# Regrouping the attention round of a fused attention, MoE and FFN kernel, with four smaller moves of waits and reads

## The chip, the cores and the metric

The kernel runs on one core of a Trainium2 chip, as one launch. The metric is device time in microseconds, the median of three runs; lower is better. TensorE (PE in the profile) multiplies, VectorE (DVE), ScalarE (ACT) and GpSimd (POOL) work on tiles, and SyncE (SP) only issues DMAs and waits.

## The reference

Three layers follow each other. The first is a gated linear attention over 4 batches of 8 heads, 768 tokens each, head size 48; the second a top-1 mixture of 8 experts; the third a dense layer with an ELU.

```
for t in range(S):                                   # attention, per batch and head
    state = alpha[t][:, None] * state + outer(k[t], v[t])
    y[t] = q[t] @ state
x = y as [3072, 384]
logits = normalised(x) @ normalised(expert_emb).T / tau
e = argmax(logits); gate = softmax(logits)[e]
x = gate * (relu(x @ w1[e]) @ w2[e])                 # w1 384x1024, w2 1024x384 per expert
h = x @ w_in                                         # 384x2048
out = where(h > 0, h, exp(min(h, 0)) - 1) @ w_out    # 2048x384
```

## The kernel before

All engines run side by side, each through its own hand-written list of steps, and each step waits on semaphores for the steps that it needs.

**Attention.** Two heads make a pair, so there are 16 pairs (PAIRS), and round n works on pair n, with parts of the pairs before and behind it. A pair has 6 chunks of 128 tokens, in two halves (0 and 1, three chunks each). `ROUND_PE`, `ROUND_VE`, `ROUND_AC` and `ROUND_PO` are the orders of a round on TensorE, VectorE, ScalarE and GpSimd; `("Tk1", 1)` in round n is the step Tk1 of pair n+1. The steps are:

- TensorE: Ta, Tk, Tq transpose alpha, k and q (three 128x128 each); KT transposes the scaled keys (3 and 2); A is the score product (12 matmuls of 48 rows, in pairs in two row halves of the array); KV the chunk states (20 matmuls with 128x64 weights, in pairs in two column halves); Yi is scores times v (12 per half, weights 128x48); Ys is q times the state (20, weights 48x48, rows and columns halved); YN transposes y and multiplies it with the expert embeddings (6 per half); CT counts tokens per expert (once in four rounds).
- VectorE: G and F are prefix scans over 768 tokens (lines 836 and 844), R a reciprocal between them; Kh and Qh scale keys and queries; M0 masks the scores of half 0; S2 to S5 (line 710) run the state recurrence over the chunks; LA adds logits. The R.., N.. and Y.. names are the router's small steps (argmax, slots, softmax, and the order of the experts), each a chain of its own.
- ScalarE: Kt, C1, Ea, Yn, Ln, yT copy out of PSUM; St1 to St5 copy the chunk states with a scale; SS and SP square x for the norm; Gq is the softmax's Exp.
- GpSimd: M1 masks the scores of half 1 (line 1007), Gm, Za, Zm are small; P0 to P8 are the inverse square root of the norms (lines 959 to 978, "roots"); SC scatters rows of x to DRAM, sorted by expert (line 1015), six per batch; U0 issues the loads of w1 of the second expert (lines 1143 and 1133, 1.5 MB each).

With PPB = 4 pairs per batch, batch b's router steps start in round 4(b+1); the lists `SLOW`, `SOON`, `LAST` hang them behind steps of a round. The last batch (PARTIAL, b = 3) is finished after round 15. PSUM has 8 banks, and each step names the bank that it uses, so the reuse of a bank is a wait.

**Experts.** Rows are processed in 31 tiles of 128 tokens, sorted by expert: XT transposes a tile, M10 and M11 are the two halves of x @ w1 (9 matmuls each), HT transposes h, M2 is h @ w2 (24). ScalarE (Xe, Re, He) and VectorE (Xe, He, Ye) copy and split operands. Tiles 0 and 1 take rows of the first three batches only (EARLY = 2). SyncE waits for all scatters of the last batch before it loads tile 2. `position(t)` reads the expert's number of tile t from `kth` into a register, once in each of M10, M11 and M2. `climb` runs a ladder of small VectorE steps that compute `row`, `kth`, `end_i` (up to n_tiles) and `dst` (to the end).

**FFN.** Six groups of 512 tokens; H is x @ w_in, O accumulates g @ w_out, 16 blocks each; E, M, G, L are the ELU and its split. The output of four tiles per group goes through `of` and four indirect DMAs (line 1406) issued by GpSimd, which also waits for their completion before the program ends.

Of the kernel before, what the change touches and what calls it, by code (L numbers as in the profile page):

```python
# [10 lines left out]
P = 128  # L11
# [59 lines left out]
def build(nc, q, k, v, alpha, emb, tau, w1, w2, w_in, w_out, out):  # L71
# [30 lines left out]
    with ExitStack() as ctx:  # L102
# [138 lines left out]
        for x in (a_at, d_at, e_at, r_at):  # L241
# [56 lines left out]
        ROUTE_PE = [({}, {"Ta0": ("CT",)})] * (BATCHES - 1) + [({"YN1": ("CT",)},)]  # L298
        ROUTE_AC = [({}, {}, {"Ln0": ("Gq",)})] * (BATCHES - 2) + [({}, {"Ln1": ("Gq",)}), ({"Ln0": ("SL0",), "Yn1": ("SL1",), "Ln1": ("Wc", "Gq")},)]
# [22 lines left out]
        def steps_pe(n):  # L322
            out_ = with_route(ROUND_PE, ROUTE_PE, n)
            if n == -1:
                out_ = [("Tk1", 0), ("Ta0", 1), ("Tq0", 0), ("Tq1", 0), ("Ta1", 1)]
            if n in (0, 1):
                out_.insert(place_of(out_, "A0") + 1, ("Tk0", n + 1))
            if n == 0:
                out_.remove(("Tk0", 2))
            return out_  # L330

        def steps_ve(n):
            out_ = with_route(ROUND_VE, ROUTE_VE, n)
# [1297 lines left out]
```

## Time and profile before

| | |
|---|---|
| median of 3 runs | 910.74 us (910.71 to 911.87) |
| the profiled execution | 911.53 us, of which 909.9 us are its span |
| PE busy | 879.2 us (97%) |
| DVE, ACT, POOL busy | 436.1, 320.5, 267.9 us |
| granted TensorE clock | 0.996 of full |

Times in the rows are microseconds from the span's start. The end of a matmul is modelled: a row of three matmuls that starts at 97.95 and lasts 0.49 has its last start some 0.27 (the length of one) before its end. What counts on TensorE is the distance from start to start. A busy TensorE is therefore not a TensorE at its peak. The span falls into attention (0 to 179.3), the hand-over to the experts and the first tiles (to 203.9), the experts (to 475.4, one tile in 9.6), the FFN (to 898.9) and an end without matmuls (to 909.9).

### The profile page before, as it was taken

How to read it: one execution, taken by the hardware profiler on the slowest of the kernel's cores; microseconds unless marked ns; L12 is line 12 of the kernel's file. 1: busy time of each engine (PE TensorE's matmuls, PEld its weight loads, DVE VectorE, ACT ScalarE, POOL GpSimd, SP SyncE). 2: the span in 40 equal slices, each digit the busy share in tenths (PEclk: the TensorE clock that was granted, in tenths of full speed). 3: DMA queues.
4: the chain of work that ended last, by engine and by line, in shares of the span. 5: the costliest groups of instructions: out<-in, count | busy, mean ns of one | idle time of the engine just before them, and what ended most of it. 6: DMA issues, size and time to landing. Idle time of an engine off the chain costs nothing. (4 is left out here: it accounts for less than half of the span.)

```text
span 909.9 us, 16294 instructions
## 1 busy us (share of the span) xinstructions
PE 879.2 (97%) x5725; PEld 777.8 (85%) x5725; DVE 436.1 (48%) x828; ACT 320.5 (35%) x709; POOL 267.9 (29%) x279
## 2 busy tenths in 40 slices
PE   8999999889999999999999999999999999999995
PEld 5787888678989989999888899999999899899894
DVE  7887888872222222322325545445445445445442
ACT  4565646623222222232332223223223223223221
POOL 3114244447545754564807201001001001001001
PEclk9999999999999999999999999999999999999998
DMA  9965774688878789746807102002002002000000
GB/s 155 163 120 116 155 151 96 212 280 268 259 243 280 246 259 302 238 137 189 220 20 235 42 1 70 1 1 70 1 1 70 1 0 70 1 1 35 1 1 35
DMA packets 140975, 107.92 MB, mean 119 GB/s; under 512 B 103354, under 2 KB 129074, under 8 KB 140898
## 3 DMA queue, kind: packets, MB, share of 16 engines
q0 software_dynamic: 25696, 66.09, 22.8%
q1 hardware_dynamic: 115202, 40.79, 20.2%
q8 instruction: 50, 0.82, 0.4%
q14 instruction: 27, 0.22, 0.1%
HBM read 89.51 MB, written 17.35 MB: 117 GB/s over the span
## 5 line engine op out<-in xcount | busy, mean ns | idle before, releaser
L1406 POOL DMA_INDIRECT out<-of,idi x24 | 23.6, 983 | 370.1 <-DVE of L1492 305.4
L1226 PE MATMUL bank<-WX,hdTh 128*128 (+1 forms) x496 | 129.5, 342 | 3.0 <-DVE hdTl L1279 1.7
L1450 PE MATMUL bank<-xT_h,wi_h 128*128 128x512 f32 x288 | 114.3, 397 | 0.0
L1450 PE MATMUL bank<-xT_l,wi_h 128*128 128x512 f32 x288 | 113.7, 395 | 0.0
L1450 PE MATMUL bank<-xT_h,wi_l 128*128 128x512 f32 x288 | 113.5, 394 | 0.0
L1532 DVE TENSOR_SCALAR em<-ee 128x512 f32<-128x512 f32 x96 | 44.7, 465 | 136.0 <-ACT ee L1510 133.8
L1510 ACT ACTIVATE ee<-bank 128x512 f32<-128x512 f32 x96 | 57.3, 597 | 147.2 <-PE bank L1450 144.2
L1212 PE MATMUL bank<-WX,xdTh 128*128 (+1 forms) x372 | 99.7, 403 | 3.3 <-ACT xdTh L1252 1.5
L1513 ACT ACTIVATE g_h<-gg 128x512 fp32r<-128x512 f32 x96 | 60.6, 632 | 116.3 <-DVE gg L1537 114.6
L1150 POOL TENSOR_TENSOR WX<-raw_w,WX 128x3072 fp32r<-128x3072 f32 x14 | 95.5, 6821 | 17.8 <-DMA WX<-moe_w 12.9
L1541 DVE TENSOR_TENSOR g_l<-gg,g_h 128x512 fp32r<-128x512 f32 x96 | 69.9, 728 | 60.2 <-ACT g_h L1513 59.3
L1226 PEld LDWEIGHTS bank<-WX,hdTh 128*128 128x128 f32 x496 | 88.2, 188 | 3.6 <-issue 3.4
L1477 PE MATMUL bank<-wo_h,g_h 128*128 128x384 f32 x380 | 82.6, 339 | 1.2 <-DVEq L423 0.6
L1226 PE MATMUL bank<-WX,hdTl 128*128 (+1 forms) x248 | 83.7, 337 | 0.0
L1212 PEld LDWEIGHTS bank<-WX,xdTh 128*128 128x128 f32 x372 | 67.6, 189 | 18.1 <-issue 4.4
L1477 PE MATMUL bank<-wo_h,g_l 128*128 128x384 f32 x380 | 81.7, 338 | 0.2 <-DVE g_l L1541 0.2
L1477 PE MATMUL bank<-wo_l,g_h 128*128 128x384 f32 x380 | 81.4, 337 | 0.0
L1477 PEld LDWEIGHTS bank<-wo_h,g_h 128*128 128x128 f32 x380 | 68.8, 188 | 10.6 <-issue 1.7
L1258 ACT ACTIVATE hdTh<-bank 128x512 fp32r<-128x512 f32 x62 | 33.8, 596 | 119.8 <-PE bank L1235 119.8
L1537 DVE SCALAR_TENSOR_TENSOR gg<-bank,em 128x512 f32<-128x512 f32 x96 | 66.4, 692 | 3.7 <-DVEq L423 0.5
L1261 ACT ACTIVATE hd<-bank 128x512 f32<-128x512 f32 x62 | 37.0, 598 | 88.5 <-PE bank L1212 88.5
L1477 PEld LDWEIGHTS bank<-wo_h,g_l 128*128 128x128 f32 x380 | 67.3, 189 | 0.5 <-DVE g_l L1541 0.5
(215 smaller groups left out, 1387.2 us busy)
## 6 DMA issues: line engine op xcount, KB each, us to landing
WX<-moe_w POOLq DMA_DIRECT2D x14, 1536.0 KB, 9.9
raw_w<-moe_w POOLq DMA_DIRECT2D x14, 1536.0 KB, 8.6
xd<-sorted_x SPq DMA_DIRECT2D x31, 193.0 KB, 5.3
sorted_y<-yd SPq DMA_DIRECT2D x31, 192.5 KB, 4.6
xg<-sorted_y SPq DMA_DIRECT2D x6, 770.0 KB, 4.4
nat_a<-alpha SPq DMA_DIRECT2D x32, 144.0 KB, 3.3
nat_k<-k SPq DMA_DIRECT2D x32, 144.0 KB, 3.5
nat_q<-q SPq DMA_DIRECT2D x32, 144.0 KB, 3.6
```

The lines of the kernel that those rows point to most:

```text
L1150: po.tensor_tensor(lower[:, cols], raw[x][:, :], upper[:, cols].bitcast(F32), ALU.subtract).then_inc(s_w, 1)
L1212: last = pe.matmul(bank[3 + i][:, :], xdT[t % 2][a][:, k * P:(k + 1) * P], WX[:, bass.ds(off + (b * WE + k * F + i * COLS), COLS)], start= ...
L1226: last = pe.matmul(y_out(t)[:, 0:DM], hdT[a][:, k * P:(k + 1) * P], WX[:, bass.ds(off + (b * WE + KD * F + k * DM), DM)], start=(k == 0 an ...
L1258: return ac.activation(hdT[0][:, cols], bank[1 + i][:, :], ACT.Copy)
L1261: return ac.activation(hd[:, cols], bank[3 + i][:, :], ACT.Relu)
L1450: last = pe.matmul(bank[4 + i % 2][:, :], a[:, k, w], b[:, k, :], start=(k == 0 and m == 0), stop=(k == KD - 1 and m == 2))
L1477: last = pe.matmul(bank[t][:, 0:DM], a[i % 2][:, t * P:(t + 1) * P], b[:, i, :], start=(i == 0 and m == 0), stop=(i == K2 - 1 and m == 2))
L1510: return ac.activation(ee[i % 2][:, :], bank[4 + i % 2][:, :], ACT.Exp)
L1513: return ac.activation(g_h[i % 2][:, :], gg[i % 2][:, :], ACT.Copy)
L1532: return ve.tensor_scalar(em[i % 2][:, :], ee[i % 2][:, :], 1.0, -1.0, ALU.min, ALU.add)
L1537: return ve.scalar_tensor_tensor(out=gg[i % 2][:, :], in0=bank[4 + i % 2][:, :], scalar=0.0, in1=em[i % 2][:, :], op0=ALU.max, op1=ALU.add)
L1541: return ve.tensor_tensor(g_l[i % 2][:, :], gg[i % 2][:, :], g_h[i % 2][:, :].bitcast(F32), ALU.subtract)
```

## The change

The order of the round changes. On TensorE, steps of one kind stand together: `KT0 KT1 Tk1`, then `A0 A1`, then the full-array steps `YN0 Ta0 Ta1 YN1 Tq0 Tq1 Tk0`, then `KV Yi0 Yi1`, `Ys0 Ys1`. KV moves from the fifth place to the thirteenth, and the states St1 to St5 on ScalarE and S2 to S5 on VectorE move to the end of the round. The banks are dealt out anew to allow it. VectorE takes both Kh before M0, and the router's small steps mostly stand behind S5. Squares (SS, SP) and Gq stand in other gaps of ScalarE. All six scatters of batch 2 move to round 14, and the router's steps that they need move too (Rp, Rr, Ng, Nk behind S5 of round 13; Ns, Nt, Nr behind Kh1 of round 14).

After round 15, GpSimd's roots come before U0 ("roots ahead of reads"). VectorE's ladder is cut at n_tiles, and Ye 0 and He 1 stand before its rest. `position` keeps what it read, and a step K reads the next tile's position before HT0. In the FFN, output tiles 0 and 2 go to ScalarE and 1 and 3 to VectorE (before: the other way round), the last group's O14 of tile 3 waits until tiles 0 and 1 of O15 are done, and SyncE waits for the last output scatters in GpSimd's place.

```diff
-        ROUND_PE = (("KT0", 0), ("A0", 0), ("KT1", 0), ("Tk1", 1), ("KV", 0), ("A1", 0), ("Ta0", 2), ("YN0", -1), ("Ta1", 2),
-                    ("Tq0", 1), ("YN1", -1), ("Tq1", 1), ("Tk0", 2), ("Yi0", 0), ("Yi1", 0), ("Ys0", 0), ("Ys1", 0))
-        ROUND_VE = (("G", 1), ("Kh0", 1), ("M0", 0), ("Kh1", 1), ("R", 1), ("S2", 0), ("S3", 0), ("S4", 0), ("S5", 0),
-                    ("F", 1), ("LA", -1), ("Qh0", 1), ("Qh1", 1))
-        ROUND_AC = (("yT0", -1), ("Kt0", 0), ("yT1", -1), ("Kt1", 0), ("St1", 0), ("St2", 0), ("St3", 0), ("St4", 0), ("St5", 0),
-                    ("Ea0", 2), ("Yn0", -1), ("Ln0", -1), ("C1", 0), ("Ea1", 2), ("Yn1", -1), ("Ln1", -1))
+        ROUND_PE = (("KT0", 0), ("KT1", 0), ("Tk1", 1), ("A0", 0), ("A1", 0), ("YN0", -1), ("Ta0", 2), ("Ta1", 2), ("YN1", -1),
+                    ("Tq0", 1), ("Tq1", 1), ("Tk0", 2), ("KV", 0), ("Yi0", 0), ("Yi1", 0), ("Ys0", 0), ("Ys1", 0))
+        ROUND_VE = (("G", 1), ("Kh0", 1), ("Kh1", 1), ("M0", 0), ("R", 1), ("F", 1), ("LA", -1), ("Qh0", 1), ("Qh1", 1),
+                    ("S2", 0), ("S3", 0), ("S4", 0), ("S5", 0))
+        ROUND_AC = (("yT1", -1), ("Kt0", 0), ("Kt1", 0), ("C1", 0), ("Yn0", -1), ("Ln0", -1), ("Ea0", 2), ("Ea1", 2),
+                    ("Yn1", -1), ("Ln1", -1), ("St1", 0), ("St2", 0), ("St3", 0), ("St4", 0), ("St5", 0), ("yT0", 0))
...
-                    out_ += [("U0", 1), ("PM", b)] + roots + [("SC", b * C + j) for j in range(C)]
+                    out_ += [("PM", b)] + roots + [("U0", 1)] + [("SC", b * C + j) for j in range(C)]
                 elif b == PARTIAL - 1 and r == 1:
-                    i = place_of(out_, "M1")
-                    out_[i:i] = roots
-                    out_ += [(f"X{i}", b) for i in range(X_STEPS)] + [("SC", b * C + j) for j in range(HC)]
+                    out_ += roots + [(f"X{i}", b) for i in range(X_STEPS)]
                 elif b == PARTIAL - 1 and r == 2:
-                    i = place_of(out_, "M1") + 1
-                    out_[i:i] = [("SC", b * C + j) for j in range(HC, C)]
+                    out_ += [("SC", b * C + j) for j in range(C)]
...
+        def a_bank(i, h):
+            return bank[(3 if i else 6) + h]
+
+        def kt_bank(i):
+            return bank[3 if i else 5]
...
             def position(t):
-                return pe.value_load(kth[0:1, t:t + 1], min_val=0, max_val=E - 1) if t >= EARLY else 0
+
+                if t not in places:
+                    k = pe.value_load(kth[0:1, t:t + 1], min_val=0, max_val=E - 1) if t >= EARLY else 0
+                    places[t] = (k, pe.snap(k % 2 * (2 * WE)) if t >= EARLY else 0)
+                    places.pop(t - 2, None)
+                return places[t]
...
-            for t in range(GT):
-                po.wait_ge(s_out[t], 16 * GROUPS)
...
+                if i == K2 - 2 and n == GROUPS - 1:
+                    return [of_tile(i, t) for t in range(GT - 1)][-1]
                 if i == K2 - 1 and n == GROUPS - 1:
...
                     for t in range(GT):
...
+                        if t == GT - 2:
+                            of_tile(K2 - 2, GT - 1)
+                        last = of_tile(i, t)
...
             for g in range(1, GROUPS):
                 sp_tokens(sp, g)
+            for t in range(GT):
+                sp.wait_ge(s_out[t], 16 * GROUPS)
...
-            climb(ve, "vector", n_emb, len(ladder))
-            d(("Ye", 0), ("He0", 1), ("He1", 1), ("Ye", 1), ("Xe", 2), ("Xe", 3))
+            climb(ve, "vector", n_emb, n_tiles)
+            d(("Ye", 0), ("He0", 1), ("He1", 1))
+            climb(ve, "vector", n_tiles, len(ladder))
+            d(("Ye", 1), ("Xe", 2), ("Xe", 3))
...
-                d(("HT0", t), ("HT1", t))
+                d(("K", t + 1), ("HT0", t), ("HT1", t))
```

## Rows read from the trace of the kernel before

**Rows 1.** Busy time by stretch: length, then PE, PEld, DVE, ACT, POOL, clock, DMA.

```profile
33.78:43.88 10.10, 9.96 (x126) 8.31 (x124) 8.26 (x15) 5.33 (x17) 1.31 (x4) 1.00 1.05 155
33.78:147.37 113.59, 110.32 (x1364) 92.11 (x1362) 91.14 (x192) 68.92 (x222) 34.70 (x75) 1.00 0.71 139
74.61:86.24 11.63, 9.96 (x126) 8.30 (x124) 8.70 (x22) 6.84 (x19) 2.79 (x10) 1.00 0.54 103
147.37:158.07 10.70, 10.52 (x130) 8.67 (x128) 9.40 (x30) 6.47 (x23) 5.93 (x14) 1.00 0.16 33
158.07:169.07 11.00, 9.15 (x116) 7.33 (x114) 9.60 (x22) 4.56 (x15) 8.20 (x10) 1.00 0.94 310
169.07:179.32 10.25, 9.27 (x121) 8.00 (x120) 8.47 (x13) 7.85 (x30) 1.51 (x3) 1.00 0.48 160
```

**Rows 2.** Timeline of TensorE in round 8: start, length, line, operands, count.

```profile
96.81 0.94 PE L615 MATMUL bank<-qh,kh 48*128 48x128 f32 x12
97.67 0.44 PE L601 MATMUL bank<-ident,kh 128*128 128x128 f32 x2
97.95 0.49 PE L590 MATMUL bank<-ident,nat_k 128*128 128x128 f32 x3
98.59 0.79 PE L625 MATMUL bank<-vn,ktsb 128*64 128x48 f32 x20
...
105.19 1.30 PE L654 MATMUL bank<-qh,std 48*48 48x128 f32 x20
106.42 0.55 PE L601 MATMUL bank<-ident,kh 128*128 128x128 f32 x3
```

**Rows 3.** Timelines of ScalarE (first row) and VectorE in round 8.

```profile
99.62 0.86 ACT L906 ACTIVATE st<-bank,gam 128x48 f32<-128x48 f32 x4
...
99.95 1.39 DVE L710 SCALAR_TENSOR_TENSOR std<-std,gam,st 128x48 f32<-128x48 f32 x4 [0.57 <-ACT st L906]
```

**Rows 4.** Timelines in round 1: VectorE's scan F and LA, GpSimd's M1.

```profile
29.29 1.76 DVE L844 TENSOR_TENSOR_SCAN inv<-al,seedF 128x768 f32<-128x768 f32 x1 [0.19 <-issue]
30.97 0.79 DVE L829 COPY LR<-LP 128x48 f32<-128x48 f32 x1
...
29.30 2.41 POOL L1007 TENSOR_SCALAR_AFFINE_SELECT asb<-asb 128x768 f32<-128x768 f32 x1 [2.40 <-ACT asb L912]
```

**Rows 5.** Timeline of ScalarE in round 6, at Gq.

```profile
80.30 1.28 ACT L892 ACT_TABLE_LOAD   x1
```

**Rows 6.** Timeline of GpSimd after round 15: U0's load, P8, the first scatter.

```profile
180.47 0.84 POOL L1143 DMA_DIRECT2D WX<-moe_w  x1 [9.58 <-DMA xd<-sorted_x]
...
185.90 0.26 POOL L978 TENSOR_SCALAR root_n<-root_t 128x6 f32<-128x6 f32 x1
...
188.45 1.83 POOL L1015 DMA_INDIRECT sorted_x<-xb,slot  x1 [2.30 <-DVE WX L725]
```

**Rows 7.** The hand-over as one stretch; last two columns: DMA share, GB/s.

```profile
182.00:200.00 18.00, 14.83 (x79) 12.47 (x78) 15.29 (x50) 6.32 (x10) 10.47 (x17) 1.00 0.98 329
```

**Rows 8.** Timelines of SyncE (first row) and TensorE from the hand-over on.

```profile
201.36 2.58 SPq L1298 DMA_DIRECT2D xd<-sorted_x  x3
...
187.53 1.64 PE L1212 MATMUL bank<-WX,xdTh 128*128 128x512 f32 x6 [1.45 <-ACT hd L1261]
...
203.88 0.55 PE L1195 MATMUL bank<-ident,xd 128*128 128x128 f32 x3
...
211.72 1.67 PE L1212 MATMUL bank<-WX,xdTh 128*128 x6 [0.36 <-issue]
...
478.78 0.61 PE L1226 MATMUL bank<-WX,hdTh 128*128 x2 [1.25 <-issue]
```

**Rows 9.** The granted clock after the last matmul; columns as in rows 1.

```profile
903.00:904.00 1.00, 0.00 (x0) 0.00 (x0) 0.00 (x0) 0.00 (x0) 0.01 (x1) 0.60 0.46 169
```

**Rows 10.** The program's last instructions on GpSimd: timeline, and line 102 (ns).

```profile
902.05 0.96 POOL L1406 DMA_INDIRECT out<-of,idi  x1 [0.30 <-issue]
...
L102 POOLq DRAIN  x1: 4813/4813/4813, 904.9 to 904.9; - x1
```

More of the change, by code:

```diff
@@ L325, in steps_pe @@
                 out_ = [("Tk1", 0), ("Ta0", 1), ("Tq0", 0), ("Tq1", 0), ("Ta1", 1)]
-            if n in (0, 1):
-                out_.insert(place_of(out_, "A0") + 1, ("Tk0", n + 1))
             if n == 0:
-                out_.remove(("Tk0", 2))
+                out_ = [("KT0", 0), ("A0", 0), ("Tk0", 1), ("KT1", 0), ("Tk1", 1), ("KV", 0), ("A1", 0), ("Ta0", 2), ("Ta1", 2),
+                        ("Tq0", 1), ("Tq1", 1), ("Yi0", 0), ("Yi1", 0), ("Ys0", 0), ("Ys1", 0)]
+            if n == 1:
+                out_.remove(("Tk1", 2))
+                i = place_of(out_, "A0") + 1
+                out_[i:i] = [("Tk0", 2), ("Tk1", 2)]
             return out_
@@ L405, in build @@
                     2, (f"H{last}",))
-        acE = Steps(sem("acE"), ["E0", "G0"] + [f"O{t}" for t in range(1, GT, 2)]
+        acE = Steps(sem("acE"), ["E0", "G0"] + [f"O{t}" for t in range(0, GT, 2)]
                     + [f"{x}{c}" for c in range(1, 4) for x in "EG"]
@@ L605, in step @@
                     if i:
-                        veA.wait(pe, "M0", n)
+                        acA.wait(pe, "C1", n - 1)
+                        acA.wait(pe, "Kt1", n)
+                        for b in range(PARTIAL):
+                            if n == round_of(b, 2):
+                                veA.wait(pe, "Rw", b)
                     else:
-                        acA.wait(pe, "C1", n - 1)
+                        acA.wait(pe, "yT1", n - 1)
                     if n == 0:
@@ L614, in step @@
                             rows = slice(DP * h, DP * h + D)
-                            last = pe.matmul(bank[3 + h][:, m * P:(m + 1) * P], kh[u][rows, c * P:(c + 1) * P],
+                            last = pe.matmul(a_bank(i, h)[:, m * P:(m + 1) * P], kh[u][rows, c * P:(c + 1) * P],
                                              qh[u][rows, c * P:(c + 1) * P], start=True, stop=True)
@@ L620, in step @@
                     pe.wait_ge(s_v[u], n // 2 * 32 + 32)
-                    acA.wait(pe, "St5", n - 1)
+                    acA.wait(pe, "Ln0", n - 1)
                     for c in range(C - 1):
@@ L637, in step @@
                         acA.wait(pe, f"yT{i}", n - 1)
-                    for b in range(PARTIAL):
-                        if n == round_of(b, 1) and i:
-                            veA.wait(pe, "Rw", b)
+                        veA.wait(pe, "M0", n)
                     for m in range(HC):
@@ L662, in step @@
                     elif i:
-                        acA.wait(pe, "Ln0", n)
+                        acA.wait(pe, "C1", n + 1)
                     else:
-                        acA.wait(pe, "St5", n + 1)
-                        acA.wait(pe, "Ln1" if n < PAIRS - 1 else "Ln0", n - 1)
-                        acA.wait(pe, "Kt1", n)
+                        acA.wait(pe, "Kt0", n + 1)
+                        acA.wait(pe, "St5", n)
                     if n == 0:
@@ L690, in pe_a @@
                     if (name, p) == ("Tk1", 0):
-                        pe.matmul(bank[3][:, 0:DM], ones[:, :], zero_row[:, 0:DM], start=True, stop=True)
+                        pe.matmul(bank[6][:, 0:DM], ones[:, :], zero_row[:, 0:DM], start=True, stop=True)
         def ve_a(ve, d):
```

124 lines of the change are left out of this document (69 added, 55 removed).

## The prediction

> **What bounds the kernel now.** I read the busy time by stretch first [rows 1]. Rounds 2 to 12 take 113.59 us, 11 rounds; a plain one is 10.10 long, with TensorE called busy for 9.96 of it and VectorE for 8.26. Busy is no proof that TensorE is the limit, so the starts in one round's timeline come next [rows 2]. Matmuls that follow in one mode of the array start 0.11 apart. Where the mode changes (full array, row halves, column halves, both) the distance is 0.20, and 0.15 to 0.21 instead of 0.11 once more behind it: A0's last matmul starts at 97.48, KT1 at 97.67; Ys's last at 106.22, KT0 at 106.42. A plain round has eight such changes. Tk1's last matmul starts at 98.17 and KV only at 98.59: it waits for the copy Kt1, 0.22 beyond the mode change. The timeline shows two smaller data waits, before YN1 (0.09) and before Tk0 (0.14). So a round of 10.09 is 9.64 of TensorE's own pace and 0.45 of waits.
>
> Special rounds come on top: CT adds 0.46 (rounds 5, 9, 13), and in round 6 the first Exp loads its table for 1.28 in front of C1 [rows 5], which with what waits for it makes that round 11.63 [rows 1]. In rounds 13 to 15 TensorE is busy for less and VectorE sets the pace (9.40 of 10.70, 9.60 of 11.00). After round 15 the chain of waits runs over DMA: 329 GB/s from 182 to 200, a DMA share of 0.98 [rows 7], and SyncE loads tile 2 only when the last scatter has landed [rows 8]. From there TensorE keeps its pace to the end of the FFN but for single holes. Behind the last matmul (898.9) 11 us remain, 4.81 of them one DRAIN on GpSimd [rows 10].
>
> **The plain round after.** Kinds stand together, so five mode changes are left of eight (KT and Tk to A, A to YN, Tk0 to KV, Yi to Ys, Ys to KT). KV with 64 columns and Yi with 48 are both column halves, so I count no change between them. Three times some 0.18 is 0.55, and TensorE alone would need 9.64 - 0.55 = 9.1. Kt1, C1 and Ea now have more work between themselves and their readers, which hides all three old waits.
>
> A new wait takes part of it back. The states come late in the round: KV's last matmul starts 6.3 behind KT0 (transposes, A, YN: 5.5; the change 0.2; KV's own 0.57). From KV's last start (98.59 + 0.79 - 0.22 = 99.16) to the end of S5 (99.95 + 1.39 = 101.34) it takes 2.18 [rows 2, 3]. Ys1 may therefore start at 6.3 + 2.18 + 0.06 = 8.55, where TensorE would be ready at 8.25; its ten starts take 0.59 and the change to KT0 0.20. That makes 9.35, and 0.75 less than now. VectorE holds it: G and F 1.75 each, Kh, M0 and Qh six times 0.47, the four S 1.3, R, LA and the waits between dependent steps 0.6, in all 8.2. A0 and A1 lie in y's banks and wait for yT1: that ends 0.6 behind KT0, A0 comes at 1.0.
>
> What the regrouping sets on top of each other is M1 and the scan F. C1 ends 3.5 behind KT0, and F runs from 3.2 to 5.0. In round 1 this happened by chance: M1 started with F, took 2.41 and ended 0.66 behind it, and VectorE's next step took 0.79 instead of 0.2 [rows 4]. After, M1 ends at 5.65; Yi1 needs it at 7.0, LA waits for Ln1 until 5.4 and loses 0.3, and S2 can't start before 7.1 anyhow. So it costs nothing under a cover of 0.4 on VectorE; without cover it would be 0.6 a round.
> The Trainium skill (SBUF — State Buffer, Who interferes with whom) says that a VectorE step with two SBUF inputs and a GpSimd step that reads SBUF exclude each other for the whole step. It speaks against this placement. By that rule, the trace agrees: 2.41 is the rest of the scan and M1's own time.
> The Trainium skill (TensorEngine Tiling (Array Packing), Key Properties) says that changing the tiling mode, not the tile, drains TensorE. It would make the three removed changes the gain, and KV to Yi free; the trace agrees with the 0.20.
>
> **Sum over attention.** Round 1: F starts earlier behind R, M1 no longer sits in front of Yi1: 1.5 less. Rounds 2 to 12: seven plain ones at 9.35 (65.4), two with CT at 9.8 (19.6), round 7 with Gq and its table load behind Kt1 where C1 isn't waiting for it, but Ns, Nt, Nr hold M0 back by 1.4: 9.7; round 11 the same without the load: 9.45. Together 104.2 against 113.6: 9.4 less. Round 13: 9.8 against 10.70. But 16 small router steps (about 0.23 each, 3.6 in all) now stand between S5 and the scan G of pair 15, which starts 2.3 into round 14 in place of 1 before it; M0, F, Qh, S2 to S5 follow in line, so round 14 becomes 12.0 against 11.00. Round 15 loses its waits for Kt1 and Ln0 and its KV stands late: 1.3 less. At attention's last matmul: 1.5 + 9.4 + 0.9 - 1.0 + 1.3 = 12.1 less.
>
> **The hand-over.** Here I expect part of it to be lost. U0 issues 3.1 MB at 180.47; after, it stands behind P8 [rows 6]. The roots themselves start early (PM needs only NM, P1 needs N1), so P8 ends 2.0 sooner than now against round 15, and U0 comes 36.9 behind the start of round 13 where it now comes 33.1: 3.7 later. What follows rides on the same engines: U0's 3.1 MB, 1.5 MB of zero rows and 1.2 MB of scatters are 5.8 MB, which is what 18 us at 329 GB/s move [rows 7]. The engines have been idle just before 182, so their end moves by the whole 3.7. The scatters lie behind U0 in one queue and land last. Tile 2 is loaded 3.3 behind them, and XT of tile 2 (203.88) comes 3.6 later against round 13. Round 13 itself starts 1.5 + 9.4 = 10.9 earlier: XT 2 at 196.6, 7.3 less than now.
> The earlier P8 lets Gq, and with it the copies that M10 of tile 1 waits for (187.53, 1.45 idle [rows 8]), come 1.05 sooner, and the cut ladder brings He0 1 and M2 1 forward by 0.7. Both end in the wait for tile 2: TensorE would stand idle there for some 5 us. Nothing of them is counted.
>
> **The holes behind.** The reads of `kth` leave two holes: before M10 of tile 3 (211.72) and M2 of tile 29 (478.78) TensorE idles for "issue" [rows 8]; with the value in a register the first shrinks by 0.6, the second by 0.8 (load, two register steps, assertion). The other 85 reads lie under running matmuls and give nothing. The swap of output tiles gives 0.2 once, at the first group.
>
> **The end.** The last group's tile 0 is done three matmuls (0.52) earlier, and with ScalarE's copy 0.07 quicker; four scatters of 1.26 each follow back to back on GpSimd and bound the end, so 0.6. GpSimd then waits for the landings until 904.65 and starts its DRAIN at 904.9 [rows 10]. With the wait on SyncE the DRAIN can start when the last issue is done, at 903.1: 1.8 less if its 4.81 is a length of its own, 0 if it counts from the landings. Its long time after everything had landed speaks for a length of its own; I take 1.7. SyncE's wait ends under the DRAIN.
>
> **Total.** 7.3 + 0.6 + 0.8 + 0.2 + 0.6 + 1.7 = 11.2. The profiled execution's 911.53 becomes 900.3, and the median, 0.8 below it, 899.5.
>
> **Rivals.**
> - The DMA isn't the limit (the queued bytes flow quicker, or U0 finds a gap): then M2 of tile 1 sets XT 2, and 12.1 + 1.75 = 13.9 is kept in place of 7.3. For it: the share of 0.98 holds some slack. Against: the landings do follow each other at full rate. 893. Chance 0.12.
> - The clock falls. Behind the last matmul (898.9) the granted clock drops to its lower level, 1.2 GHz, within the stretch 903 to 904 [rows 9], 4 to 5 us into the idle time, and I expect an idle time of 3.3 to 5.5 before XT 2. Full matmuls at half pace would cost up to 3.5 until it rises; I take 2.5: 902. Chance 0.2.
> - The round shrinks less, to 9.8 (KV to Yi is a change, F or LA collide more often): 12 x 0.45 = 5.4 back: 905. Chance 0.12.
> - Slower: M1 under F blocks VectorE on its longest line. If F's followers come late enough that S2 starts 1 us behind St2, each of rounds 1 to 13 costs 0.95 more; from a plain round of 10.3 on, the total is at or above today's. It needs S2 to be held until 8.1 where I see VectorE free at 6.7. 912 to 915. Chance 0.06.
> - The regrouping doesn't shorten the round at all (as many stalls at the new borders): then the hand-over's 3.6 against the holes and the end, 3.9, gives 910.4, no change. Chance 0.04.
>
> My own case has 0.46, with 896.5 to 902.5 as its own range. The range over all is 893 to 905.5. A measurement of this kernel tells about 0.2% (1.8 us) from nothing. Faster 0.90, same 0.04, slower 0.06.
>
> **What would show it.** Right: plain rounds of 9.3 to 9.4; Ys1 waiting for S5; five distances of 0.20 a round; M1 at 2 us; round 14 near 12; the last scatter landing 3.7 later against round 13 and an idle TensorE of some 5 us before XT 2; the clock there; a DRAIN of 4.8 that starts with the last issue. Wrong: a plain round bound by VectorE or by yT1, or scatters that land as before.

## Result, and the profile after

The change takes 907.59 us (median of 6 runs, 907.17 to 909.92) where the kernel before takes 910.73 (6 runs): ratio 0.9967, 95% interval 0.9956 to 0.9979. That is 3.1 us less where 11.2 were forecast; the range ended at 905.5. The profiled execution took 907.89, its span is 906.1. The rounds and the end came out near the forecast; the hand-over to the experts didn't.

First the rounds, as stretches (columns as in [rows 1]): a plain round, rounds 2 to 12, round 8, round 14, round 15.

```profile
51.26:60.58 9.32, 9.20 (x126) 8.12 (x124) 7.77 (x18) 6.58 (x21) 2.54 (x5) 1.00 0.65 126
32.62:137.70 105.08, 102.09 (x1364) 90.17 (x1362) 93.41 (x192) 68.81 (x218) 50.39 (x75) 1.00 0.77 152
89.35:99.26 9.91, 9.20 (x125) 8.11 (x124) 8.30 (x18) 6.58 (x21) 7.47 (x9) 1.00 0.89 213
147.49:159.40 11.91, 8.74 (x117) 7.27 (x115) 10.22 (x30) 5.27 (x18) 8.61 (x11) 1.00 0.78 268
159.40:171.38 11.98, 11.85 (x120) 10.48 (x119) 7.07 (x12) 6.75 (x26) 2.12 (x3) 0.72 0.44 150
```

The plain round is 9.32 (10.10 in [rows 1]; forecast 9.35), round 14 is 11.9 (forecast 12.0). Rounds 2 to 12 together are 0.9 longer than forecast, and the third row says where: round 8, and round 12 like it, at 9.91. The last row is the surprise. TensorE is called busy for 11.85 of 11.98, yet the granted clock is 0.72: it stood at its lower level, 1.2 GHz, from 159.3 to 166.2, and again from 200.3 to 207.1. Such a stretch is called a fall below. Its level in three stretches (the clock is third from the right):

```profile
159.40:166.10 6.70, 6.70 (x43) 6.14 (x41) 3.49 (x5) 2.59 (x9) 2.12 (x3) 0.50 0.56 207
200.40:207.10 6.70, 3.87 (x10) 2.90 (x11) 0.56 (x1) 0.49 (x1) 3.39 (x3) 0.50 0.65 154
166.30:200.30 34.00, 25.67 (x187) 21.92 (x186) 23.10 (x67) 13.75 (x34) 11.82 (x18) 1.00 0.55 187
```

TensorE's timeline ahead of the first fall and in it:

```profile
152.75 0.85 PE L606 MATMUL bank<-ident,nat_q 128*128 128x128 f32 x6 [0.72 <-DVE lsum L837]
153.52 0.79 PE L646 MATMUL bank<-vn,ktsb 128*64 128x48 f32 x20
154.14 1.48 PE L662 MATMUL bank<-asb,vn 128*48 128x128 f32 x24
157.58 0.64 PE L673 MATMUL bank<-qh,std 48*48 48x128 f32 x8 [1.96 <-DVE std L731]
158.61 0.86 PE L673 MATMUL bank<-qh,std 48*48 48x128 f32 x12 [0.39 <-DVE std L731]
159.40 1.33 PE L618 MATMUL bank<-ident,kh 128*128 128x128 f32 x5
160.65 2.93 PE L636 MATMUL bank<-qh,kh 48*128 48x128 f32 x24
```

It idled for 0.72, 1.96 and 0.39 in round 14, each time for VectorE; the A steps then take 2.93 for the 24 matmuls that took 1.61 before.

Round 8 shows the other loss: VectorE's scan F, then on GpSimd the scatters of the second half and M1 (L1028).

```profile
92.52 1.76 DVE L865 TENSOR_TENSOR_SCAN inv<-al,seedF 128x768 f32<-128x768 f32 x1
...
91.34 0.99 POOL L1036 DMA_INDIRECT sorted_x<-xb,slot  x1 [0.17 <-issue]
92.64 2.40 POOL L1036 DMA_INDIRECT sorted_x<-xb,slot  x1 [0.30 <-issue]
95.34 0.96 POOL L1036 DMA_INDIRECT sorted_x<-xb,slot  x1 [0.30 <-issue]
96.31 0.88 POOL L1028 TENSOR_SCALAR_AFFINE_SELECT asb<-asb 128x768 f32<-128x768 f32 x1
```

One issue takes 2.40 in place of 0.96: it begins 0.12 behind the scan F (92.52 to 94.27) and ends 0.8 behind its end. M1 comes at 96.31, 7.0 behind the round's start where a plain round has 3.6, and Yi1 waits 0.7 for it.

Now the hand-over: GpSimd (P8, U0's two transfers, first scatter), a VectorE step beside them, SyncE, TensorE at tile 2, and the stretch of [rows 7].

```profile
177.23 0.28 POOL L999 TENSOR_SCALAR root_n<-root_t 128x6 f32<-128x6 f32 x1
179.12 0.89 POOL L1164 DMA_DIRECT2D WX<-moe_w  x1 [1.60 <-issue]
180.02 0.77 POOL L1154 DMA_DIRECT2D raw_w<-moe_w  x1
181.10 1.87 POOL L1036 DMA_INDIRECT sorted_x<-xb,slot  x1 [0.30 <-issue]
...
179.37 3.52 DVE L746 TENSOR_TENSOR WX<-raw_w,WX 128x768 fp32r<-128x768 f32 x4
...
178.91 8.36 SPq L1344 DMA_DIRECT2D sorted_x<-zero_row  x8
200.03 2.58 SPq L1323 DMA_DIRECT2D xd<-sorted_x  x3
...
202.44 0.90 PE L1220 MATMUL bank<-ident,xd 128*128 128x128 f32 x3 [7.25 <-DMA xd<-sorted_x]
...
182.00:200.00 18.00, 12.16 (x71) 11.19 (x69) 10.12 (x33) 3.27 (x6) 5.97 (x6) 1.00 0.86 315
```

U0 goes out at 179.1, 41.4 behind round 13 (33.1 before, forecast 36.9). XT of tile 2 starts at 202.44, only 1.4 sooner than in [rows 8], after 7.25 of idle TensorE, and the second fall of the clock lies right there. Behind it the small parts, answering to [rows 8] and [rows 10]:

```profile
211.41 1.64 PE L1236 MATMUL bank<-WX,xdTh 128*128 x6
477.63 0.61 PE L1249 MATMUL bank<-WX,hdTh 128*128 x2 [0.50 <-PEq L430]
...
900.11 0.96 POOL L1431 DMA_INDIRECT out<-of,idi  x1 [0.31 <-issue]
...
L102 POOLq DRAIN  x1: 7594/7594/7594, 898.3 to 898.3; - x1
```

The hole ahead of tile 3's M10 is gone, that ahead of tile 29's M2 is 0.50 in place of 1.25. M10 of tile 3 is still only 0.31 earlier than before (211.41 for 211.72): nearly all that was gained by 137.7 (9.67) is spent by there, and 3.5 of the span's 3.8 come from behind it. The DRAIN's record now begins while the last scatters are still to be issued; it ends at 905.9, 4.8 behind the end of the last issue (901.07). Before, it ended 6.7 behind.

### The profile page after: what moved, and what is told of

It is laid out like the page before. It is cut to its first block and busy times, and to the rows that moved or that the text cites. A ratio compares the mean times of both kernels' runs of the same rounds, so it can differ in the third digit from the quotient of the medians.

```text
span 906.1 us, 16135 instructions
## 1 busy us (share of the span) xinstructions
PE 873.0 (96%) x5725; PEld 779.2 (86%) x5725; DVE 438.0 (48%) x828; ACT 321.8 (36%) x709; POOL 286.5 (32%) x279
## 3 DMA queue, kind: packets, MB, share of 16 engines
q1 hardware_dynamic: 115202, 40.79, 20.1%
## 5 line engine op out<-in xcount | busy, mean ns | idle before, releaser
L1431 POOL DMA_INDIRECT out<-of,idi x24 | 26.8, 1116 | 366.3 <-ACT of L1537 303.1
L1171 POOL TENSOR_TENSOR WX<-raw_w,WX 128x3072 fp32r<-128x3072 f32 x14 | 95.6, 6826 | 15.6 <-DMA WX<-moe_w 11.2
L1510 PEld LDWEIGHTS bank<-wo_h,g_h 128*128 128x128 f32 x376 | 68.0, 188 | 10.7 <-ACTq L430 1.3
L1299 DVE TENSOR_TENSOR xdTl<-bank,xdTh 128x384 fp32r<-128x384 f32 x31 | 17.3, 557 | 113.4 <-ACT xdTh L1277 113.4
## 6 DMA issues: line engine op xcount, KB each, us to landing
xd<-sorted_x SPq DMA_DIRECT2D x31, 193.0 KB, 5.0
```

The lines of the kernel that those rows point to most:

```text
L1171: po.tensor_tensor(lower[:, cols], raw[x][:, :], upper[:, cols].bitcast(F32), ALU.subtract).then_inc(s_w, 1)
L1510: last = pe.matmul(bank[t][:, 0:DM], a[i % 2][:, t * P:(t + 1) * P], b[:, i, :], start=(i == 0 and m == 0), stop=(i == K2 - 1 and m == 2))
```

## The experiments

The kernel before ran beside every set, since its level differs between them: its median was 922.0 in the first set, 922.5 in the second, 911.4 in the third, 913.6 in the fourth and 923.6 in the fifth. The record names chips 15, 9, 6, 13 and 13: the last two sets have the same number and lie 10 apart, so the level isn't shown to be a property of a chip. Between sets only ratios, or distances within one trace, are set beside each other. The changed kernel ran again in the second set alone, and stands at 0.985 there. Each run has one trace; its time needn't be the median.

**e1: U0 ahead of the roots again.**

```diff
-                    out_ += [("PM", b)] + roots + [("U0", 1)] + [("SC", b * C + j) for j in range(C)]
+                    out_ += [("U0", 1), ("PM", b)] + roots + [("SC", b * C + j) for j in range(C)]
```

> The changed kernel with one thing undone: U0 (3.1 MB of expert 1) is issued ahead of PM and the roots again. Theory (the late U0 sets the last landing): xd 0 and 1 landed at 169.2, so U0 goes out at about 170.2 in place of 179.1, 3.1 MB are through before the zero rows and scatters start, the last of which lands at about 190 in place of 199.2. XT 2 then stands right behind M2 of tile 1 (194.9), so at 195.1 in place of 202.4 (-7.3), with no idle time there and no second fall of the clock (-2.0 more): some 898.5, 9 below the changed kernel. Rival 1 (the zero rows and scatters are slow by themselves, in their queues): last landing still near 197 to 199 and the time at 906 or above. Rival 2 (U0 now delays PM and the roots on GpSimd, or the first tiles' loads): P8 ends later than 177.5 by 2 or more, XT 2 near 198, 901 to 903.

Measured: 901.35, ratio 0.9781 (0.9768 to 0.9795) against 0.9850 for the changed kernel in the second set, at a like level (below). U0 and XT 2:

```profile
173.26 0.84 POOL L1164 DMA_DIRECT2D WX<-moe_w  x1 [8.91 <-DMA xd<-sorted_x]
...
197.56 0.55 PE L1220 MATMUL bank<-ident,xd 128*128 128x128 f32 x3 [1.01 <-DMA xd<-sorted_x]
```

XT 2 stands 57.5 behind round 13 in place of 64.7, and the idle time is 1.0. This trace has no fall in round 15, which is part of that difference. Two other runs of the set, e3 and e4, have none there either and U0 late: their XT 2 stands 64.2 and 62.9 behind round 13, and their medians are 5.9 and 7.8 above e1 (each has a fall elsewhere). So the theory holds, though the last landing came later than I had said (SyncE could load tile 2 at 195.0, where I had 190 for the landing), which is why 1.0 is left. P8 ends 17.2 behind the start of round 15, 0.6 later than in e3, so the second rival has a small part; its range, 901 to 903, holds the time.

**e2: the kernel before, with U0 late.** The same two lines, the other way round.

> The kernel before with one thing of the change: U0 is issued behind P8 in place of ahead of PM. Theory (the late U0 sets the last landing and the wait lets the clock fall): U0 goes from 180.5 to about 186.5 (P8 ends up to 1 earlier than 185.9), the last landing and XT 2 follow by 4.5 to 6, 208.5 to 210; TensorE is idle there for over 5 us more, the clock falls and costs 2: 915 to 918, 4.5 to 7.5 above the kernel before. Rival (the order of U0 means nothing, all bytes share the engines anyhow): 910 to 912.

Measured: 931.94, ratio 1.0108 (1.0092 to 1.0123): 10 lost, more than the forecast 4.5 to 7.5.

```profile
198.07 0.89 POOL L1143 DMA_DIRECT2D WX<-moe_w  x1 [1.29 <-issue]
...
221.64 0.90 PE L1195 MATMUL bank<-ident,xd 128*128 128x128 f32 x3 [6.50 <-DMA xd<-sorted_x]
```

XT 2 is 43.2 behind the start of round 15; it is 36.1 in g_without_rounds (below), where the level is like and U0 stands first. So the place of U0 costs 7 by itself. The clock is at its lower level for 10.2 from 218.3, and from XT 2 to M10 of tile 3 it takes 10.6 where the kernel before takes 7.8: that is the rest. e1 and e2 together show the place of U0 from both sides.

**e3: the wait for tile 2 filled.**

```diff
-            d(("M11", 1), ("M2", 0), ("HT0", 1), ("HT1", 1), ("M2", 1), ("XT", 2))
+            d(("M11", 1), ("M2", 0), ("HT0", 1), ("HT1", 1), ("M2", 1))
+            for _ in range(9):
+                pe.matmul(bank[6][:, 0:DM], ones[:, :], zero_row[:, 0:DM], start=True, stop=True)
+            d(("XT", 2))
```

> The changed kernel with nine matmuls of no use (ones by zeros, 384 columns, some 0.65 each) between M2 of tile 1 and XT of tile 2, so that TensorE isn't idle in the 7.6 us before XT 2. Theory (the clock falls because of that idle time and that costs time): no lower level from 200.3 to 207.1; XT 2 stays at 202.4; M10 of tile 3 at 209.3 to 209.6 in place of 211.4; the time 2.0 less, 905.5. Rival (the clock falls anyhow, or what follows is bound by weights or copies): M10 of tile 3 within 0.5 of 211.4, time 907 to 907.6.

Measured: 907.23, ratio 0.9853 (0.9830 to 0.9875), no better than the changed kernel's 0.9850. The stretch from XT 2 to M2 of tile 2, in e3 and then in the changed kernel:

```profile
204.28:215.99 11.71, 10.67 (x54) 8.41 (x53) 2.50 (x4) 3.80 (x8) 9.45 (x4) 1.00 1.03 303
```
```profile
202.44:215.93 13.49, 12.45 (x53) 9.73 (x54) 2.50 (x4) 3.80 (x8) 9.44 (x4) 0.82 1.01 292
```

The second fall costs 1.8 where it lies. But in e3 the clock had already fallen at 194, in M2 of tile 1, for 3.4, and with the nine matmuls behind it XT 2 comes 3.35 behind its load's issue in place of 2.41. Part of the 1.8 is given back there, and the time shows none of it.

**e4: round 14 filled.**

```diff
+                    if (name, p) == ("YN1", PAIRS - 3):
+                        veA.wait(pe, "Qh1", PAIRS - 2)
+                        for _ in range(1):
+                            pe.matmul(bank[0][:, 0:DM], ones[:, :], zero_row[:, 0:DM], start=True, stop=True)
+                    if (name, p) == ("Yi1", PAIRS - 2):
+                        veA.wait(pe, "Kh0", PAIRS - 1)
+                        for _ in range(2):
+                            pe.matmul(bank[1][:, 0:DM], ones[:, :], zero_row[:, 0:DM], start=True, stop=True)
```

> The changed kernel with three matmuls of no use in round 14: one ahead of Tq0 of pair 15, two behind Yi1 of pair 14, where TensorE idles for 0.7 and 2.0. Theory (the idle time of round 14 lets the clock fall at 159.3, and round 15 runs at half pace for 6.8 us on the path to the hand-over): no lower level from 159.3 to 166.2, KV of pair 15 at 163.2 in place of 166.35, N1, P8, U0 and the last landing each about 3 sooner, XT 2 at 199.4 in place of 202.4, the time 904.5. Rival (round 15 is bound by VectorE and ScalarE, so the clock costs little): the lower level gone and KV within 1 of 166.35, time above 906.5. Rival 2: the clock falls all the same, and nothing changes (907.6).

Measured: 909.10, ratio 0.9857 (0.9841 to 0.9872). No lower level in round 15, which is 9.70 long (from KT0 to the start of YN's last matmul, as every length of round 15 below; the changed kernel's is 11.87); it fell at 193.0 and at 203.2 instead, and nothing is gained. e1 and e3 had no fall in round 15 either, without this filling, so this run alone settles nothing. It led to k1 to k3.

**c_after_again and g_without_rounds.** The changed kernel unedited, as the measure; and the kernel before with only the positions, the cut ladder, the output tiles' swap and the end.

> The changed kernel itself, unedited, as the measure for the other runs of this chip (the chip of the last four runs had the kernel before at 922.0 in place of 910.7). If this chip is like the first one: 907.6, the clock at its lower level twice. If it is like the second: the kernel before at 922, this one near 909 (the other variants of it gave 907.2 and 909.1 there), rounds 8 and 12 at 11.0 and no fall in round 15.

> The kernel before with all of the change but the attention part: positions read ahead of the waits, the ladder cut in two, output tiles swapped and two of the last group's steps reordered, landings awaited by SyncE; steps of the rounds, banks, roots, scatters and U0 as before. Theory (the holes and the end gave what was forecast, all that was lost lies ahead of tile 3): against the kernel before -0.6 (tile 3), -0.8 (M2 of tile 29), -0.2, -0.6 and -1.8 (DRAIN), 3.9 in all, ratio 0.9957; the regrouping with the late U0 then gave nothing on the first chip. Rival (the holes only move, the DRAIN counts from the landings): -1.5 or less, ratio 0.9984 or more.

Measured: 909.05, ratio 0.9850 (0.9836 to 0.9863), two falls as in the first trace, here of 10.2 each; and 916.40, ratio 0.9939 (0.9924 to 0.9953). g's forecast of 0.9957 is just outside its interval, on the good side: the small parts give their 3.9 or more. If they give as much beside the first result, where the whole change gives 3.1, regrouping and late U0 together gave nothing to speak of there. The traces also say where the old round loses at the level of 922: in g rounds 7, 8, 11 and 12 take 10.8, 11.9, 14.7 and 11.2, together 8.2 of some 11 (a fall lies in round 11), and in e2 they lose 9.1. The new round loses less there (10.65 for round 8 in c_after_again). All four rounds hold scatters; why the level differs wasn't tried.

**f_scatters_last and h.** Scatters behind the round.

```diff
                 elif b < PARTIAL - 1 and r == 4:
-                    i = place_of(out_, "M1")
-                    out_[i:i] = [("SC", b * C + j) for j in range(HC, C)]
+                    out_ += [("SC", b * C + j) for j in range(HC, C)]
```

> The changed kernel with the three scatters of the second half of batches 0 and 1 (rounds 8 and 12) at the end of GpSimd's round in place of ahead of M1. Theory (rounds 8 and 12 are long because a scatter's issue under F takes 2.4 and holds up M1): both rounds 9.35 (9.80 with CT not in them) in place of 9.91, 1.1 less than the changed kernel where it shows 9.91; M1 in round 8 starts 3.5 behind KT0. Rival (those rounds are long because the loads of q, k and alpha land late beside the scatters): no gain, or a loss of up to 1 where the scatters' later packets meet the next loads.

> Both: U0 ahead of PM and the roots again, and the three scatters of rounds 8 and 12 at the end of GpSimd's round. Theory: the two are independent, so the sum: -7.8 (as e1 stood to the changed kernel's estimate of 909 on its chip) and -1.1 against the changed kernel on the same chip, 8.5 to 9. Rival (the earlier attention end meets the last landing, which doesn't come earlier): as e1 alone, -7.8.

Measured: 910.96, ratio 0.9872 (0.9857 to 0.9887), and 902.56, ratio 0.9784 (0.9770 to 0.9799). No gain. M1 starts on time in both (93.3), so its part is right, but rounds 8 and 12 of f take 11.0 and 10.9, no less than in c_after_again (10.65 and 10.58), now with Ys0 waiting 0.6 for the states. Round 9 of h takes 12.95, for 6.8 of which the clock is at its lower level. Whether the late scatters cause either isn't shown. h's sum of both gains is missed; its rival, as e1 alone, holds.

**b1 and b4.** Two more suspects, one at a time in the changed kernel: the cast W2 ahead of the masks in round 15, and the second of U0's transfers behind the scatters.

```diff
-                out_ = [("M0", n), ("M1", n), ("W2", 0)] + sums + [("W0", 0), ("LA", n - 1), ("W1", 0),
+                out_ = [("W2", 0), ("M0", n), ("M1", n)] + sums + [("W0", 0), ("LA", n - 1), ("W1", 0),
```
```diff
-                    out_ += [("PM", b)] + roots + [("U0", 1)] + [("SC", b * C + j) for j in range(C)]
+                    out_ += [("PM", b)] + roots + [("U0", 1)] + [("SC", b * C + j) for j in range(C)] + [("U1", 1)]
...
```

> The changed kernel with the cast W2 (1.75 on VectorE) first in round 15's list in place of behind M0 and M1, where VectorE idles for 4 us. Theory (round 15 is 10.3 even without a fall of the clock, since W2 stands between the masks and the sums S2 to S5, and Ys0 waits 1.0 for S2): Ys0 0.2 behind Yi1 in place of 1.0, round 15 at 9.3 to 9.4 where the clock holds, everything up to XT 2 earlier by 1.0; the ratio to the kernel before 0.984 where the unedited one has 0.985 (second chip), 906.6 where that has 907.6 (first chip). Rival (A0, YN and the states' path set round 15, or only the clock does): no change in round 15 beyond 0.2.

> The changed kernel with the second of U0's two transfers (1.5 of its 3.1 MB) issued behind the six scatters in place of ahead of them. Theory (the bytes ahead of the last scatter and zero row set XT 2): 1.57 MB at 329 GB/s are 4.8 us, so the last landing that tile 2 needs, and XT 2, come 4 to 4.8 earlier against round 13 (64.7 and 66.2 with the change on the two chips: 60 to 61.4), TensorE waits there for 2.5 or less; 4 to 6 less in all, ratio 0.979 to 0.981 on the second chip. Rival 1 (the issue of scatters and zero rows on their engines sets the end): XT 2 at most 1 earlier. Rival 2 (the late half of expert 1's weights is then missed): XT 2 earlier, but a new wait of 3 or more at tile 3, and the time as before.

Measured: 907.38, ratio 0.9956 (0.9941 to 0.9970), and 909.19, ratio 0.9966 (0.9954 to 0.9978); the changed kernel has 0.9967. W2 moved to 158.46 and nothing followed: round 15 stays at 11.81, at the lower clock. With the fall in it b1 alone doesn't decide on W2; k2, with W2 in its place and round 15 at 8.78, does, and my theory on W2 falls. b4 misses too: XT 2 stands 65.2 behind round 13.

```profile
180.30 0.90 POOL L1166 DMA_DIRECT2D WX<-moe_w  x1 [1.62 <-issue]
181.50 1.76 POOL L1038 DMA_INDIRECT sorted_x<-xb,slot  x1 [0.31 <-DVE WX L746]
...
190.08 0.80 POOL L1156 DMA_DIRECT2D raw_w<-moe_w  x1
...
202.87 0.90 PE L1222 MATMUL bank<-ident,xd 128*128 128x128 f32 x3 [6.52 <-DMA xd<-sorted_x]
```

Counted from U0 the last landing came 17.4 later in place of 20.1, so 2.7 earlier, not 4.8. The moved half then ran beside tile 2's load: XT 2 follows that load's issue (198.52) by 4.3 in place of 2.4. Swapping the bytes within this stretch gives nothing to speak of.

**b2 and b3: the remedies together.** b2 has U0 first, and W2 and W0 ahead of the masks. b3 has besides one scatter ahead of M1 and two behind it:

```diff
-                    out_[i:i] = [("SC", b * C + j) for j in range(HC, C)]
+                    out_[i:i + 1] = [("SC", b * C + HC), out_[i]] + [("SC", b * C + j) for j in range(HC + 1, C)]
```

> Both remedies: U0 ahead of PM and the roots, and W2 and W0 first in round 15. Theory: e1's gain and 1.0 more, ratio 0.977 on the second chip (e1 had 0.978), 898.5 or less on the first. Rival (as in e1 the landing sets XT 2 and the landing hangs on U0, not on round 15): as e1.

> As the run before, and in rounds 8 and 12 one scatter ahead of M1 and two right behind it in place of three ahead. Theory: M1 starts with C1's end (3.5 behind KT0) and takes 2.0 under F as in the other rounds, rounds 8 and 12 lose 0.5 each where they are at 9.91 (first chip); on the second chip, where they are at 10.6 to 11.0 for another reason, 0 to 0.3 each: ratio 0.9765 to 0.977. Rival: the later scatters make Yn0 of round 9 wait for their landing, round 9 above 9.9.

Measured: 899.04, ratio 0.9867 (0.9852 to 0.9881), and 896.68, ratio 0.9842 (0.9829 to 0.9854). b2 stands 8.3 below b1 in the same set. It differs from it by U0's place and by W0; W0 wasn't tried by itself, so U0's place has the 8.3 only as far as W0 gives nothing. b3 takes rounds 8 and 12 to 9.32. Its hand-over (round 8, U0, XT 2):

```profile
89.84:99.17 9.33, 9.20 (x126) 8.12 (x124) 7.78 (x18) 6.58 (x21) 7.15 (x9) 1.00 0.92 225
...
170.43 0.84 POOL L1164 DMA_DIRECT2D WX<-moe_w  x1 [6.81 <-DMA xd<-sorted_x]
...
194.98 0.49 PE L1220 MATMUL bank<-ident,xd 128*128 128x128 f32 x3
```

XT 2 follows M2 of tile 1 without a wait, the second fall is gone with the idle time, in b2 as well, and this is the shortest time found: 10.7 below b1 and 14.7 below the kernel before, in one set. By ratio e1 and h stand lower (0.978), at the level of 922, where this version wasn't run.

**k1, k3, k2: the clock.** k1 is b3 with e4's three matmuls, k3 with four; k2 is the changed kernel with e4's and e3's filling and one more ahead of M2 of tile 1.

> The last version (U0 first, W2 and W0 first, scatters split one and two) with three matmuls of no use in round 14: one ahead of Tq0, two behind Yi1. Theory (the idle time of round 14 lets the clock fall, and the fall costs round 15 some 2.5): no lower level between 157 and 168, round 14 at 11.9, round 15 at 9.3 to 9.4 in place of 12.3, and 3 less by the end: 893.7, ratio 0.981 where the version without has 0.9842. Rival (the clock falls all the same, somewhere): 896 to 897.5.

> As the run before with three in place of two matmuls behind Yi1, so that next to no idle time is left ahead of Ys0 (0.65 each, 2.0 idle). Theory: if two leave enough idle time for the fall, three don't: as told for the run before, 893.7 to 894. If both hold the clock, this one is equal or 0.3 later. Rival: the fall stays, 896 to 898.

> The changed kernel with every long idle time of TensorE filled: three matmuls of no use in round 14, one ahead of M2 of tile 1, nine ahead of XT 2. Theory (two falls together cost what the changed kernel lost beside the late U0): no lower level before the end; round 15 at 9.7 to 10.3 in place of 11.9, XT 2 at 200.5 to 201, M2 of tile 2 11.7 behind XT 2 in place of 13.5; the time 3 to 4 below the changed kernel, ratio 0.9925 to 0.9935 where that has 0.9967. Rival (the lateness of U0 holds everything, the clock is hidden behind it): 0.995 or more.

Measured: 901.17, ratio 0.9860 (0.9845 to 0.9876); 900.44, ratio 0.9861 (0.9842 to 0.9880); 905.01, ratio 0.9896 (0.9881 to 0.9912). Round 15 and XT 0 in k3, then round 15 and XT 2 in k2:

```profile
158.39:167.30 8.91, 8.79 (x119) 7.67 (x117) 7.30 (x12) 6.70 (x26) 4.31 (x4) 1.00 0.43 156
...
170.19 0.55 PE L1228 MATMUL bank<-ident,xd 128*128 128x128 f32 x3 [2.74 <-DMA xd<-sorted_x]
```
```profile
159.49:168.70 9.21, 8.94 (x119) 7.67 (x117) 7.21 (x12) 7.00 (x27) 2.12 (x3) 1.00 0.54 178
...
176.13 0.89 POOL L1172 DMA_DIRECT2D WX<-moe_w  x1 [1.61 <-issue]
...
200.04 0.55 PE L1228 MATMUL bank<-ident,xd 128*128 128x128 f32 x3 [2.05 <-DMA xd<-sorted_x]
```

All three have round 15 at 8.78 to 8.79, the forecast's 8.7, k2 with W2 where the change puts it; the changed kernel has 11.87. So the fall costs round 15 3.1. In the changed kernel the gain reaches tile 2: U0 3.0 sooner, XT 2 2.4 sooner, the ratio 0.9896 in place of 0.9967, better than the forecast 0.9925 to 0.9935. The forecast that no lower level is left misses: one lies from 202 to 206. k1 and k3 miss their 0.981, and their rival holds. XT 0 waits for its load until 170.19, U0 waits for the same loads, M2 of tile 0 starts at 184.5 as in b3, and XT 2 waits 2.2 and 1.8 for its load, where it waited for nothing in b3. A loss that counts in one version is hidden behind a transfer in the next.

**k5 and k6: U0 without that wait.** k1 and b3, with this taken out (U0's weights go elsewhere than the tiles):

```diff
-                    for t in range(EARLY):
-                        po.wait_ge(s_xd[t], 16)
```

> As k1 (U0 first, W2 and W0 first, scatters one and two, round 14 filled), but U0 doesn't wait for the loads of the first two tiles. Theory (these waits hold GpSimd until 171.4, U0 until 172.3 and with them PM, P8 and tile 1's copies): U0 at about 167.3, PM at 169.4 in place of 173.9, P8 at 173.4; the 3.1 MB share the engines with the loads of tiles 0 and 1, which land 1 to 2 later, XT 0 at 171 to 172; M2 of tile 0 at 181 to 182 in place of 184.5, XT 2 at 192 to 193; 4 less than k1, ratio 0.981 to 0.982. Rival (tiles 0 and 1 come 4 or more later, behind 3.1 MB): M2 of tile 0 at 184 or later, ratio 0.986 or more.

> As k5 without the matmuls of no use: round 15 at half pace again (12.3), so W1 ends near 170 and U0 gains 1 to 1.5 on b3 only (170.4). Theory: M2 of tile 0 at 183.5 to 184.5, ratio 0.983 to 0.9845; k5 below k6 by 1 to 3. Rival (the clock means nothing even with the hand-over free): k5 and k6 within 0.5.

Measured: 907.07, ratio 0.9834 (0.9809 to 0.9860), and 904.56, ratio 0.9798 (0.9783 to 0.9813), at a level where e1 has 0.9781. Nothing is gained, and both forecasts of the ratio miss. In k5 U0 goes out at 168.3, 4.9 behind the start of round 15 (14.0 in k1), and XT 0 follows at 177.97 after an idle time of 4.99, its load having run beside the 3.1 MB: 14.5 behind the start of round 15 where k1 has 11.9. That is 2.6 later, of the 4 that the rival named. k5 should have been 1 to 3 below k6 and is 2.5 above it; both have falls in the rounds (k5 in round 13, which takes 11.35, k6 around 102), so the two don't settle what the filling is worth.

**m1: two changes of the mode more.**

```diff
-        ROUND_PE = (("KT0", 0), ("KT1", 0), ("Tk1", 1), ("A0", 0), ("A1", 0), ("YN0", -1), ("Ta0", 2), ("Ta1", 2), ("YN1", -1),
+        ROUND_PE = (("KT0", 0), ("KT1", 0), ("A0", 0), ("Tk1", 1), ("A1", 0), ("YN0", -1), ("Ta0", 2), ("Ta1", 2), ("YN1", -1),
```

> The changed kernel with Tk1 between A0 and A1 in place of ahead of A0: two changes of the array's mode more in each round from 2 on. Theory (a change costs 0.2 in place of 0.11 and 0.05 to 0.1 once more behind it, so some 0.18, and the round is TensorE's pace plus the late states): a plain round 9.32 + 0.36 = 9.68, attention's end 4 to 4.5 later, the same at XT 2, ratio 1.001 to 1.002 where the changed kernel has 0.9967. Rival (the round is set by VectorE's 8.2 and the waits for S2 and S5, so that there is slack for two changes): 9.32 to 9.4, ratio as the changed kernel. Rival 2 (A1 now comes late, and with it C1, M1 and Yi1): above 9.9.

Measured: 915.73, ratio 0.9919 (0.9903 to 0.9936), 0.7% above the changed kernel's 0.9850, where 0.5% was forecast; it has a third fall, from 200 to 204. The plain round and its TensorE, then the changed kernel's:

```profile
52.00:61.67 9.67, 9.54 (x125) 8.17 (x123) 8.03 (x18) 6.58 (x21) 2.79 (x5) 1.00 0.67 123
...
52.70 0.94 PE L636 MATMUL bank<-qh,kh 48*128 48x128 f32 x12
53.56 0.55 PE L606 MATMUL bank<-ident,nat_k 128*128 128x128 f32 x3
54.04 0.94 PE L636 MATMUL bank<-qh,kh 48*128 48x128 f32 x12
```
```profile
52.28 1.61 PE L636 MATMUL bank<-qh,kh 48*128 48x128 f32 x24
```

9.67 for 9.32: 0.175 a change, as forecast (0.18). So there is no slack for two changes, which speaks for TensorE and the late states as what sets the round, and against VectorE's 8 us.

## Why the prediction was wrong, by its own steps

- **The plain round: right.** 9.32 for 9.35, Ys1 starts 0.39 behind Ys0's last matmul in place of 0.10, waiting for S5, and m1 shows that a change of the mode costs what the prediction said. M1 under F does cost nothing (forecast), taking 1.96.
- **Rounds 8 and 12: a term left out, 1.1.** The prediction weighed M1 against F, but not a scatter's issue against F: 2.40 in place of 0.96, with M1 queued behind it. b3 gives it back. The issue began 0.12 behind the scan (92.64, 92.52); in c_after_again it began 0.15 ahead of it, and took 0.96:

```profile
93.04 0.96 POOL L1036 DMA_INDIRECT sorted_x<-xb,slot  x1 [0.30 <-issue]
...
93.19 1.76 DVE L865 TENSOR_TENSOR_SCAN inv<-al,seedF 128x768 f32<-128x768 f32 x1
```

- **The hand-over: the step that failed.** "U0 comes 36.9 behind the start of round 13": it came 41.4. The forecast puts P8's end there and U0 at once behind it. P8 ended 3.0 later against round 15, by the fall just named, and U0 came 1.6 behind P8, a term put at nothing. Between the two the list has only waits long over, the read of the expert's number and the address; that it is the read is argued and not shown (in b4 the same read ahead of the second transfer, behind a scatter's issue, leaves no gap). XT 2 was forecast at 196.6 and came at 202.44: 0.9 from rounds 2 to 12, 0.3 from what lies ahead of them, 3.0 and 1.6 make 5.8. That the end of the DMA follows U0 one to one held: 23.3 from U0 to XT 2 (forecast 23.2, before 23.4).
- **The clock at tile 2: the rival had it** ("up to 3.5; I take 2.5"): 1.8 on top. With the 5.8, that makes the 7.6 that are missing at tile 3. Its condition, an idle time of 3.3 to 5.5, was passed: it was 7.25.
- **What the prediction did not ask** is what U0 in its old place would do in the new kernel. It called the hand-over's 3.6 a loss of the change. With U0 back in front the time is 5.9 and 7.8 shorter (e1 against e3 and e4), and 8.3 shorter with W0 moved too (b2 against b1).
- **The holes and the end: right.** M2 of tile 29 0.75 (forecast 0.8), tile 3's hole gone, last scatter 1.94 sooner, the DRAIN 1.9 (1.7), its 4.8 a length of its own.

The cause of the first fall is likely, but not settled. Of the five kernels with filled idle time in round 14 none had it; of the twelve others with the new rounds (the changed kernel twice, b1 to b4, f and m1; against e1, e3, h and k6) eight had it. The second set (c_after_again and f against h) and the fifth (m1 against k6) hold both kinds without filling, so the set alone doesn't decide it. In e1, e3 and h round 15 took 10.3 at the full level, for another reason: in e1 VectorE's mask starts 2.4 behind A0 where it is 1.0 in k2, and no row says why.

## What to carry to other kernels

Follow the last transfer that a stall waits for back to its issue, and ask what stands ahead of that issue in its engine's queue now: moving 3.1 MB of prefetch behind some small steps cost 6 to 8 us, most of the 8.5 that eleven rounds had gained. A fall of the clock may follow stalls that a change creates (8 of 12 kernels here, 0 of 5 where the stalls were filled), so the length of the stretch behind such stalls is to be given at both levels. And price every instruction that a VectorE scan will cover on GpSimd, the issues of scatters among them.

## What was not expected of the hardware

- A scatter's issue on GpSimd took 2.40 in place of 0.96 when it began just behind a VectorE scan of 1.76, and 1.41 when it began 1.12 behind it (c_after_again): both ended 0.8 behind the scan's end. A plain transfer's issue under a VectorE step with two SBUF inputs took 0.77.
- The clock stayed at its lower level through round 15 while TensorE was busy there for 6.70 of 6.70; in like kernels such a stay lasted from 3.4 to 10.2.
- Every kernel with filled idle time still had a fall elsewhere ahead of the end (e3: 194; e4: 193 and 203; k1: 172 and 200; k3: 172; k2: 202; k5: 140 and 178).
- The same kernel took 910.7 in one set and 922 in others, and 913.6 and 923.6 in two sets under one chip number. Rounds of the old kind were up to 4.6 longer at the higher level (a fall lies within that one); the changed kernel's round 8 lost 0.7 (10.65 for 9.91). The change is worth 0.33% at the one level and 1.5% at the other.
